# A decayed linear attention with two feed-forward layers on one core: changes of order in the scan, and the compact score array laid out with kept tokens first and heads last

## The reference

```python
for t in range(S):                      # r, k, v, w: (2, 8, 768, 48), u: (8, 48)
    cur = einsum('bhd,bhe->bhde', u * kt, vt)
    y[t] = einsum('bhd,bhde->bhe', rt, state + cur)
    state = wt[..., None] * state + einsum('bhd,bhe->bhde', kt, vt)
x = y as (2, 768, 384)
xn = (x - mean) / sqrt(var + 1e-6) * g_ln
x = x + relu(xn @ w_ch1) @ w_ch2        # 384 -> 1536 -> 384
h = relu(x @ w_in)                      # 384 -> 1024, halves u and v
v_n = (v - mean) / sqrt(var + 1e-6)
out = (u * (w_spatial @ v_n + b)) @ w_out
```

## Time and profile before

| | |
|---|---|
| profiled execution | 453.11 us |
| its span in the trace | 451.3 us |
| TensorE matmul busy | 419.4 us (93%) |
| DVE busy | 219.9 us (49%) |
| ACT busy | 148.1 us (33%) |
| POOL busy | 124.6 us (28%) |
| chain that ended last, share | PE 80%, DVE 8%, issue 7%, POOL 2% |

### The profile page before, as it was taken

How to read it: one execution, slowest core, us unless ns; L and a number is a source line. 1 busy time by engine, 2 the same in 40 slices (tenths; PEclk the granted TensorE clock), 3 DMA queues, 4 the chain that set the end, 5 groups by cost and what they waited for, 6 DMA issues and landing times.

```text
span 451.3 us, 12778 instructions
## 1 busy us (share of the span) xinstructions
PE 419.4 (93%) x5460; PEld 391.2 (87%) x5460; DVE 219.9 (49%) x492; ACT 148.1 (33%) x327; POOL 124.6 (28%) x149
## 2 busy tenths in 40 slices
PE   2998498889989999999999989999999999999997
PEld 2888388878989999999999988999998988999897
DVE  1777266673837576665744344324127754412120
ACT  3234232434334242324234341222225732111112
POOL 3656237343553432422322232001003410000000
PEclk9999769989999999999999999999999999999999
DMA  7823314322331311000000020000042200010102
GB/s 206 250 66 98 87 40 123 87 77 61 100 108 54 108 44 48 20 20 3 3 3 1 2 71 0 1 1 0 0 134 76 71 0 1 0 55 0 54 17 87
DMA packets 26556, 24.62 MB, mean 55 GB/s; under 512 B 1666, under 2 KB 23426, under 8 KB 26500
## 3 DMA queue, kind: packets, MB, share of 16 engines
q1 hardware_dynamic: 26500, 23.80, 17.8%
HBM read 21.44 MB, written 2.36 MB: 53 GB/s over the span
## 4 chain that ended last, share of the span: by engine, by line
PE 80%; DVE 8%; issue 7%; POOL 2%; ACT 1%; DMA 1%; SPq 0%; DVEq 0%; POOLq 0%; ACTq 0%
PE bank L1178 12%; PE bank L1180 10%; PE bank L1179 10%; PE low_bank L1097 6%; PE low_bank L1178 6%; PE low_bank L1180 5%; PE low_bank L1179 5%; PE high_bank L1178 3%; PE high_bank L1180 3%; PE high_bank L1179 3%; PE bank L1222 3%; PE bank L1145 2%; PE low_bank L1067 2%; PE bank L1172 2%; DVE near L843 2%
## 5 line engine op out<-in xcount | busy, mean ns | idle before, releaser
L539 POOL TENSOR_TENSOR kin<-kin,wtot 128x256 f32<-128x256 f32 x60 | 46.5, 782 | 58.4 <-PE low_bank L1097 56.5
L1097 PEld LDWEIGHTS low_bank<-rin,kin 64*64 64x64 f32 x2048 | 36.9, 140 | 15.0 <-issue 10.8
L1097 PE MATMUL low_bank<-rin,kin 64*64 64x32 f32 x2048 | 41.5, 225 | 8.9 <-DVE near L843 4.3
L800 DVE TENSOR_TENSOR rin<-rin,wtot 128x256 f32<-128x256 f32 x60 | 35.7, 603 | 27.5 <-PE low_bank L1097 27.1
L549 POOL TENSOR_TENSOR ffw<-stage,ffw 128x384 fp32r<-128x384 f32 (+1 forms) x26 | 29.2, 1123 | 44.0 <-ACT ffw L622 43.9
L843 DVE COPY_PREDICATED near<-msk,low_bank 128x256 f32<-128x256 int32 x64 | 32.7, 555 | 0.4
L1222 PE MATMUL bank<-idt 128*128 128x128 f32 x200 | 31.0, 308 | 0.0
L931 DVE SCALAR_TENSOR_TENSOR h10l<-bank,h10h 128x384 fp32r<-128x384 f32 x24 | 13.3, 555 | 31.0 <-ACT h10h L678 31.0
L1222 PEld LDWEIGHTS bank<-idt 128*128 128x128 f32 x200 | 26.9, 212 | 1.0
L556 POOL TENSOR_TENSOR vrstd<-vmv,half 128x1 f32<-128x1 f32 x12 | 7.7, 642 | 70.8 <-DVE vmv L1016 70.8
L1178 PE MATMUL bank<-xnT0h,ffw 128*128 128x384 f32 x66 | 24.8, 376 | 2.0 <-DVE h10l L931 1.8
(11 more groups left out here) (241 smaller groups left out, 1155.3 us busy)
## 6 DMA issues: line engine op xcount, KB each, us to landing
stage<-in_w SPq DMA_DIRECT2D x12, 384.0 KB, 3.4
kin<-in_kT SPq DMA_DIRECT2D x12, 256.0 KB, 3.9
rin<-in_rT SPq DMA_DIRECT2D x12, 256.0 KB, 4.3
win<-in_wT SPq DMA_DIRECT2D x12, 256.0 KB, 3.7
vin<-in_v SPq DMA_DIRECT2D x12, 192.0 KB, 4.0
out<-ob SPq DMA_DIRECT2D x12, 192.0 KB, 1.9
stage<-in_w_in SPq DMA_DIRECT2D x4, 384.0 KB, 3.3
x<-in_w_sp SPq DMA_DIRECT2D x4, 384.0 KB, 4.5
```

Of the source, the lines that this page charges most:

```text
L539: last = gp.tensor_tensor(k, k, wr[:, :, :, None].to_broadcast([P, NPR, m, c]), ALU.mult)
L800: last = ve.tensor_tensor(r, r, wl[:, :, :, None].to_broadcast([P, NPR, m, c]), ALU.mult)
L1097: mm = te.matmul(dst[s0:s0 + Q, NPR * e + a, :], kin[i % 4][lo:hi, a, s0:s0 + Q], r[:, :, 1, :], start=True, stop=True)
```

## The change

`N_KEEP` goes from 5 to 3. `near` becomes [128, 64 tokens, 8 heads]; selects read PSUM with the head as the innermost index, and `place_near` reads `near` back across it. `load_w` runs one tile further ahead. `own_term` and `own_select` of tile s + 1 move into slot (s, 3). In slot 0 `near_level(0, 0)` comes ahead of `own_term(0)`. ACT places blocks before near, and runs one small activation ahead of all else. DVE's decays, `decay_state`, `next_state` and `h1_lo` change places.

```diff
-N_KEEP = 5
+N_KEEP = 3
-        near = [place(f"near{q}", [P, H, Q]) for q in range(2)]
+        near = [place(f"near{q}", [P, Q, H]) for q in range(2)]
@@ sync
             for k, s, j in slots_of_scan():
+                if j == 0 and 4 <= s + 3 < NT:
+                    load_w(s + 3)
                 if j == 0 and 4 <= s + 2 < NT:
-                    load_w(s + 2)
                     load_k(s + 2)
                     load_r(s + 2)
@@ gpsimd, k_left
+                if i == n == 0:
+                    pool.wait_ge(uk_ready, 1)
@@ gpsimd: the memset of half comes first and raises half_set
@@ scalar, place_near (its wait for y_done or score_zeroed moves to place_blocks)
-                    last = sc.copy(score[s0:s0 + Q, :, s0:s0 + Q], near[i % 2][s0:s0 + Q, :, :])
+                    last = sc.copy(score[s0:s0 + Q, :, s0:s0 + Q], near[i % 2][s0:s0 + Q, :, :].rearrange("p t h -> p h t"))
@@ scalar
+            act.wait_ge(half_set, 1)
+            sc.activation(first_use[:, :], half[:, :], ACT.Identity, scale=half[:, 0:1])
             own_k(0)
...
                 if j == 2 and s >= 1:
+                    place_blocks(s - 1, 6)
                     place_near(s - 1)
-                    place_blocks(s - 1, 6)
@@ vector, r_right
+                if i == n == 0:
+                    dve.wait_ge(own_done, 1)
@@ vector, own_select
                 dve.wait_ge(own_done, i + 1)
-                dve.wait_ge(low_done, N_LOW * i + 1)
-                if i > ALONE:
-                    level_done(dve, i - 1, N_LOW)
                 mk = msk[:, N_MASKED * Q // 2:]
-                ve.copy_predicated(near[i % 2][:, :, :], mk[:, None, :].to_broadcast([P, H, Q]),
-                                   low[:, :, Q:2 * Q]).then_inc(own_placed, 1)
+                ve.copy_predicated(near[i % 2][:, :, :], mk[:, :, None].to_broadcast([P, Q, H]),
+                                   low[:, :, Q:2 * Q].rearrange("p h t -> p t h")).then_inc(own_placed, 1)
@@ vector, select
+                if n == N_LOW - 1 and i + 1 < NT:
+                    dve.wait_ge(own_done, i + 2)
                 src = low[:, :, 0:Q // 2] if n < N_LOW else upper_bank(i, n)
                 mk = msk[:, n * Q // 2:(n + 1) * Q // 2]
+                dst = near[i % 2][:, :, :].rearrange("p (m two c) h -> p m two c h", two=2, c=c)[:, :, 1, :, :]
                 m = Q // (2 * c)
+                if c == 1 or m == 1:
+                    dst = dst[:, :, 0, :] if c == 1 else dst[:, 0, :, :]
+                    src = src.rearrange("p h t -> p t h")
+                    mb = mk[:, :, None].to_broadcast([P, Q // 2, H])
+                else:
+                    src = src.rearrange("p h (m c) -> p m c h", c=c)
+                    mb = mk.rearrange("p (m c) -> p m c", c=c)[:, :, :, None].to_broadcast([P, m, c, H])
@@ vector, decay_plan from (2, 0) on
-                at_slot = N_LOW * s + j
-                for i in range(4, NT, 2):
-                    n = at_slot - (N_LOW * (i - 2) + 3)
-                    if 0 <= n < NL:
-                        return [(i, n)]
-                return []
+                if s % 2:
+                    return [(s + 1, n) for n in {2: (1, 2), 3: (3,)}.get(j, ())] if 3 <= s < NT - 1 else []
+                early = [(s, n) for n in {2: (4, 5), 3: (6,)}.get(j, ())] if 4 <= s < NT else []
+                return early + ([(s + 2, 0)] if j == 3 and s + 2 < NT else [])
@@ vector
-                if j == 0 and s < NT:
-                    own_select(s)
+                if k == 0:
+                    own_select(0)
                 if s < NT:
                     select(s, j)
+                if j == 3 and s + 1 < NT:
+                    own_select(s + 1)
...
+                if j == 1 and s >= 2 and carries(s - 2):
+                    next_state(s - 2)
+                n = f1_of(k)
+                if n is not None:
+                    h1_lo(n)
+                for i, m in decay_plan(s, j):
+                    decays(i, m)
                 if j == 0 and s >= 2:
                     for part in range(3):
                         x_stats(s - 2, part)
-                    if carries(s - 2) and not first(s - 2):
-                        decay_state(s - 2)
                 if j == 1 and s >= 2:
                     norm(s - 2)
+                if j == 2 and s >= 2 and carries(s - 1) and not first(s - 1):
+                    decay_state(s - 1)
...
@@ tensor, own_term (its waits for low_placed and blocks_placed are gone), near_level
+                if n == 0 and i:
+                    te.wait_ge(low_placed, N_LOW * i)
+                    te.wait_ge(own_placed, i + 1)
@@ tensor
                 if s < NT:
-                    if j == 0:
-                        own_term(s)
                     near_level(s, j)
+                    if k == 0:
+                        own_term(0)
+                    if j == 3 and s + 1 < NT:
+                        own_term(s + 1)
```

More of the change, by code:

```diff
@@ L84, in rwkv_moe_kernel @@
         half = sb("half", [P, 1])
+        first_use = sb("first_use", [P, 1])
         bias_hl = sb("bias_hl", [2, S], F32R)
@@ L211, in rwkv_moe_kernel @@
         chunk_in_sbuf = [sem(f"chunk_in_sbuf{q}") for q in range(2 + X_SLOTS)]
+        half_set = sem("half_set")
         near_zeroed = sem("near_zeroed")
@@ L556, in inv_std @@
                 gp.tensor_tensor(dst[:, i:i + 1], src[:, i, 1:2], half[:, :], ALU.pow).then_inc(std_ready, 1)
+            gp.memset(half[:, :], -0.5).then_inc(half_set, 1)
             gp.memset(near[0][:, :, :], 0.0).then_inc(near_zeroed, 1)
@@ L562, in _ @@
             gp.memset(wide[:, :, :], 0.0).then_inc(wide_zeroed, 1)
-            gp.memset(half[:, :], -0.5)
             for k, s, j in slots_of_scan():
@@ L644, in place_blocks @@
                     act.wait_ge(low_placed, N_LOW * (i + 1) + n - N_LOW + 1)
+                if i:
+                    act.wait_ge(y_done, i)
+                else:
+                    act.wait_ge(score_zeroed, 1)
                 for s0 in range(0, P, 2 * c):
@@ L829, in select @@
                     level_done(dve, i - 1, N_LOW + n)
+                if n == N_LOW - 1 and i + 1 < NT:
+                    dve.wait_ge(own_done, i + 2)
                 src = low[:, :, 0:Q // 2] if n < N_LOW else upper_bank(i, n)
                 mk = msk[:, n * Q // 2:(n + 1) * Q // 2]
-                dst = halves(near[i % 2][:, :, :], c)[1]
+                dst = near[i % 2][:, :, :].rearrange("p (m two c) h -> p m two c h", two=2, c=c)[:, :, 1, :, :]
                 m = Q // (2 * c)
[L834 to L839, removed]
-                else:
-                    src = src.rearrange("p h (m c) -> p h m c", c=c)
-                    mb = mk.rearrange("p (m c) -> p m c", c=c)[:, None, :, :].to_broadcast([P, H, m, c])
+                if c == 1 or m == 1:
+                    dst = dst[:, :, 0, :] if c == 1 else dst[:, 0, :, :]
+                    src = src.rearrange("p h t -> p t h")
+                    mb = mk[:, :, None].to_broadcast([P, Q // 2, H])
+                else:
+                    src = src.rearrange("p h (m c) -> p m c h", c=c)
+                    mb = mk.rearrange("p (m c) -> p m c", c=c)[:, :, :, None].to_broadcast([P, m, c, H])
                 ve.copy_predicated(dst, mb, src).then_inc(low_placed if n < N_LOW else middle_placed, 1)
@@ L971, in _ @@
                     select(s - 1, N_LOW + j)
-                for i, n in decay_plan(s, j):
-                    decays(i, n)
+                if j == 1 and s >= 2 and carries(s - 2):
[5 more added lines that the diff above has]
+                    decays(i, m)
                 if j == 0 and s >= 2:
@@ L976, in _ @@
                         x_stats(s - 2, part)
-                    if carries(s - 2) and not first(s - 2):
-                        decay_state(s - 2)
                 if j == 1 and s >= 2:
-                    if carries(s - 2):
-                        next_state(s - 2)
                     norm(s - 2)
+                if j == 2 and s >= 2 and carries(s - 1) and not first(s - 1):
+                    decay_state(s - 1)
                 if j == 3 and s >= 2:
                     turned_lo(s - 2, "XT", (s - 2) // TG, (s - 2) % TG)
[L985 to L989, removed]
+                if n and n % NF == 0:
+                    add_f2(n // NF - 1)
             for part in range(3):
@@ L1059, in own_term @@
                 te.wait_ge(uk_ready, i + 1)
[L1060 to L1063, removed]
                 for a in range(NPR):
@@ L1076, in near_level @@
                     k_ready(te, i, n - 1)
+                else:
+                    k_loaded(te, i)
+                    r_loaded(te, i)
+                if n == 0 and i:
+                    te.wait_ge(low_placed, N_LOW * i)
+                    te.wait_ge(own_placed, i + 1)
+                if n == 1 and i == 0:
+                    te.wait_ge(own_placed, 1)
                 if 1 <= n < N_LOW:
                     te.wait_ge(low_placed, N_LOW * i + n)
```

(2 more changed lines are left out.)

## The result

The changed kernel takes 458.6 us against 454.5; the ratio is 1.009 (95% interval 1.006 to 1.012). In a second set it is 460.4 against 454.9, 1.012 (1.009 to 1.015). The forecast was -15.6 us; the change is +4 to +6.

What follows compares the result with a forecast made beforehand. TensorE bounds the kernel; only the first 145 us, with idle time and half clock, can win. Terms -6.5 - 4.0 - 1.0 - 6.5 + 5.0 - 2.6 = -15.6 from 453.1 give 437.5, stated as 439 for the median; range 433 to 451.

Steps and rivals of the forecast that it cites:

- The gap for w: Ahead of slot 12's K turn: loading w earlier removes TensorE's 6.5 us gap, and 4.0 us of slow clock behind it.
- ACT's order: Slots 14, 22, 26, 30: blocks before near makes cast, POOL and TensorE 1.24 us later each, +5.0; +10 with slow ACT.
- one such fall: Slots 22 and 26, waiting 2.2 us in a row: one fall of TensorE's clock called likely, a loss of 1.7 us.
- The price of the strided copy: ACT's place_near reading SBUF with 32 B between elements: taken as 616 ns for each of two, twice that the other end.
- The selects: DVE reading PSUM 512 B apart: all six level selects at 0.43 us, 2.8 us a tile against 3.2; slow end 4.5.
- Rival 1: DVE reads heads slowly from PSUM: +8, so 447 us; with ACT slow too 452; chance 25%.
- Rival 2: Only ACT reads slowly, in the copy of near: +5, so 444 us; chance 15%.
- h1_lo earlier: From 88 to 145 us: h1 lower half ahead of decays and statistics saves TensorE's waits for h10l and a select, -2.6 us.
- The tile walk: Tile 4's four slots walked with own term and own select moved: 14.47 us becomes 12.1; -6.5 over tiles 0 to 4.
- start, tiles, filler and the first feed-forward slots: Start -1.0 us, tiles 0 to 4 with fewer identity matmuls -6.5, h1 lower half from 88 to 145 us -2.6.
- The signs that it named: Trace marks, such as full clock from 40 to 60 us if right, level selects at 0.73 us in every form if wrong.
- Rival 4: Fewer identity matmuls leave TensorE idle more, so its clock falls in the scan: 12 slow slots give 460 us; chance 7%.

Runs made afterwards that it cites:

- near_first: The changed kernel with ACT's old order, place_near ahead of place_blocks: 442.7 us, 0.974 of the kernel before.
- both_undone: The changed kernel with both ACT's old order and the old heads-first layout of near: 440.5 us, 0.970 of the kernel before.
- w_early_alone: The kernel before with load_w one tile further ahead and nothing else: 441.9 us, 0.973 of the kernel before.

## Why the prediction was wrong, step by step

*The gap for w: right, a little small.* Forecast -10.5 (gap and slow clock), measured alone -12.7.

*ACT's order: the right place and the right way, the wrong size; this is the step that failed.* The prediction wrote "+1.24 x 4 = +5.0. With the slow ACT end +10", and took the fast copy. In the kernel before it costs 4.9, in the changed one with the old layout 5.4, and in the kernel as changed 17.7. Two things were left out of the term. The copy's price is no term of its own but multiplies this one: 2.3 us behind the blocks instead of 1.24. And the clock fell behind each of the four waits that result, 2.7 to 4.6 us in a row. The prediction allowed "one such fall" of 1.7 us; four came, of 2.4, 3.0, 3.0 and 1.7 us. It had the earlier trace rows, a fall behind 3.20 us with 1.21 us of work in it, and did not hold its own waits against that row.

*The price of the strided copy.* It said "I take 616; twice that is the other end". It is 1151 ns, nearly the other end. Here the sentence of the Trainium skill (SBUF — State Buffer, Specifications (TRN2); the prediction cites it under Terms) that full bandwidth wants two hits in a line of 16 bytes agrees with ACT's 1151 ns, where each read has a line of its own, and there was no row to set against it.

*The selects: right.* "Fast end: all six at 0.43": measured 435 ns in each form. The cacheline rule for PSUM in the Trainium skill (PSUM — Partial Sum Buffer, Specifications (TRN2)), which the page states for matmuls, does not show in DVE's reads here. Rival 1, which had DVE slow, falls. Rival 2, ACT alone slow, had the condition right and the price wrong: "+5, so 444", where 460.4 was measured, because it added the copy to the order where the two multiply.

*h1_lo earlier: wrong sign.* The forecast was -2.6 in the slots where TensorE waited for it, and those waits did go (near_first has none for an h1 from 88 to 145 us). But in j = 3 the same move puts `turned_lo` behind an h1 that comes late: +5.5 over the tiles from slot 20 on. The prediction said of the time after 145 us that the change "can only lose, if an engine that now keeps up no longer does", and then looked for no such engine.

*The tile walk: too kind.* It gave 12.1 us for tile 4 and took -1.8 a tile. In the kernel after, that tile's level 0 starts at 64.70 and the next one's at 78.36, 13.7 us, against 14.47 before. By slots 2.5, 2.5, 3.7 and 5.0 against the walk's 2.5, 1.9, 2.8 and 4.9: the ends were right, the two middle slots not. There DVE is slower beside POOL. Two rows of the kernel after:

```profile
68.02 1.03 DVE L809 TENSOR_TENSOR rin<-rin,wtot 128x256 f32<-128x256 f32 x1
70.94 1.15 DVE L888 TENSOR_SCALAR xn<-x,mv,rstd 128x384 f32<-128x384 f32 x1 [0.42 <-POOL rstd L561]
```

They take 0.42 and 0.47 us elsewhere in this trace; both started here while POOL was in a weight half of 1.0 us. The prediction had a row of this kind and charged some 0.6 us a tile for all of it (2.4 walked, 1.8 taken).

*All other edits together.* both_undone is 14.4 us below the kernel before, w_early_alone 12.7: 1.7 more. With the 5.5 of h1_lo taken out the other edits gain 7.2 us, where start, tiles, filler and the first feed-forward slots had been put at 10.1. No run divides these 7.2 us.

Put together: 454.9 - 12.7 (w) - 7.2 (other edits) + 5.5 (h1_lo) = 440.5; + 5.4 (order) + 2.2 (layout) + 12.3 (both together) = 460.4. The forecast had -10.5, -10.1 and +5.0 for the same. That the sum comes out is no test: the 7.2 and the 12.3 are differences of the measured corners. What was measured by itself is w, h1_lo (on top of near_first), order and layout. Why ACT reads with a stride at half its rate and DVE does not is not settled.

*The signs that it named.* Of the signs of being right, the wait in front of the decays of slot 11 is gone and the table load begins at 0.73 us; the clock is not full from 40 to 60 us, and tile 4 takes 13.7 us and not 12 to 13. The waits of the last levels, 4.63, 3.44 and 3.24, reach beyond its "2 to 3.5", and `score<-near` is above 1 us. Neither of its signs of being wrong appeared: the selects are fast, and one slice only of the first 88 us is below 0.9. But for the wait of 4.63 us the loss came behind 88 us, where it had set no sign for the clock.

Rival 4, the clock, came nearest to the time (460, at 7%), but its mechanism was wrong: the clock fell behind ACT's late cast, and putting the filler back did not bring the time down (461.0).

## What to carry to other kernels

An instruction on an in-order engine that waits early for a late count makes everything behind it late: look for the wait that is stronger than it need be (here one count for two halves), before weighing the order of what feeds it. When a step is moved out of an engine's idle time into the path, its price is its length as changed by the same edit, and the wait that results has to be held against the clock: here every wait of 3.31 us or more cost another 1.7 to 3.0 us of clock, waits between 2.0 and 3.3 us did so in some cases and not in others, and those from 1.0 to 1.6 us cost nothing. And where an engine serves two consumers in one slot, serve first the one whose input is already there.

## What was not expected of the hardware

A predicated copy on DVE that reads PSUM with a stride of 512 B takes 435 ns for 256 elements, as fast as reads in a row. The slow form before (0.71 to 0.75 us) is the one that writes runs of 4 or 8 B to SBUF; no run changed the writes alone. A copy on ACT that reads SBUF with a stride of 32 B takes 1.13 to 1.18 us for 512 elements against 0.62 for reads in a row.
